# Sparse attention and two feed-forward layers on one core: the row maxima one tile later, their store between the transfers of a head, and two transfers issued by ScalarE

## The reference

```
scores = q @ k.T * (1 / sqrt(64))
thresh = max(scores, axis=-1) - tau
scores = where(scores >= thresh, scores, -1e9)
attn   = exp(scores - max(scores)) / (sum + 1e-9)
out    = attn @ v
# then x = (x @ w_a) * (x @ w_b) @ w_out; softmax-gated layer norm; @ w_out2
```

## Time and profile before

| | |
|---|---|
| median of 3 runs | 1073.68 us |
| the profiled execution | 1070.69 us, span 1068.4 us |
| attention with its prologue | about the first 388 us of the span |
| PE busy | 994.5 us (93%), 5844 matmuls |
| DVE, ACT, POOL busy | 534.7, 418.2, 251.7 us |
| PE waiting for the operands of `scores` | 49.2 us, 29 waits |
| `max_turn`: DVE waiting for POOL | 15.6 us, 16 waits |

### The profile page before, as it was taken

How to read it: one execution, slowest core, us unless ns; L and a number is a source line. 1 busy time by engine, 2 the same in 40 slices (tenths; PEclk the granted TensorE clock), 3 DMA queues, 4 the chain that set the end, 5 groups by cost and what they waited for, 6 DMA issues and landing times.

```text
span 1068.4 us, 16656 instructions
## 1 busy us (share of the span) xinstructions
PE 994.5 (93%) x5844; PEld 939.3 (88%) x5844; DVE 534.7 (50%) x863; ACT 418.2 (39%) x739; POOL 251.7 (24%) x242
## 2 busy tenths in 40 slices
PE   5789978888888889999999999999999999999998
PEld 5788878878888879999999999999999978888886
DVE  6666666666666575442122122222223485666564
ACT  2666666666666675331121121211212422322231
POOL 2656665665566670000000000000000000000000
PEclk9999999999999999999999999999999999999999
DMA  6554555555545425421001001000002200000000
GB/s 165 129 136 116 134 136 129 128 134 123 128 115 130 105 74 155 140 68 30 1 1 29 0 0 29 0 0 0 0 0 79 79 10 20 29 20 20 20 30 29
DMA packets 51566, 71.31 MB, mean 67 GB/s; under 512 B 14552, under 2 KB 24920, under 8 KB 51536
## 3 DMA queue, kind: packets, MB, share of 16 engines
q1 hardware_dynamic: 51536, 70.94, 25.2%
HBM read 33.25 MB, written 5.32 MB: 36 GB/s over the span
## 4 chain that ended last, share of the span: by engine, by line
PE 68%; SPq 9%; DMA 9%; issue 7%; DVE 3%; ACT 2%; POOL 1%; DVEq 0%; POOLq 0%; ACTq 0%
PE PS L1124 9%; PE PS L1125 9%; PE PS L1126 9%; DMA ops<-qk_lo 8%; PE PS L1195 5%; PE PS L1196 5%; PE PS L1194 5%; PE PS L1070 3%; PE PS L1253 3%; PE PS L1255 3%; PE PS L1254 3%; PE PS L1229 3%; PE PS L1227 3%; PE PS L1228 3%; PE PS L1072 2%
## 5 line engine op out<-in xcount | busy, mean ns | idle before, releaser
L1070 PE MATMUL PS<-ops 128*128 128x288 f32 x642 | 191.5, 318 | 63.3 <-DMA ops<-qk_lo 49.2
L528 POOL TENSOR_TENSOR p_lo<-prob,p_hi 128x576 fp32r<-128x576 f32 x144 | 207.3, 1440 | 135.9 <-ACT p_hi L607 130.2
L1070 PEld LDWEIGHTS PS<-ops 128*128 128x128 f32 x642 | 128.2, 200 | 78.0 <-issue 34.9
L1124 PE MATMUL PS<-x_hi,w_ab_rolled 128*128 128x384 f32 x576 | 192.5, 334 | 1.4 <-issue 1.4
L1126 PE MATMUL PS<-x_hi,w_ab_rolled 128*128 128x384 f32 x576 | 192.4, 334 | 0.0
L1125 PE MATMUL PS<-x_lo,w_ab_rolled 128*128 128x384 f32 x576 | 192.4, 334 | 0.0
L1072 PE MATMUL PS<-ops 128*128 128x288 f32 x642 | 184.3, 307 | 0.0
L944 DVE TENSOR_TENSOR gate<-gate,PS 128x384 f32<-128x384 f32 x72 | 39.9, 554 | 254.2 <-ACT gate L708 254.2
L827 DVE TENSOR_REDUCE neg_max<-PS 128x1 f32<-128x576 f32 x144 | 108.3, 754 | 107.9 <-PE PS L1072 107.8
L708 ACT ACTIVATE gate<-PS 128x384 f32<-128x384 f32 x72 | 35.5, 493 | 269.3 <-PE PS L1126 269.2
L600 ACT ACTIVATE prob<-PS 128x576 f32<-128x576 f32 x144 | 93.2, 647 | 94.6 <-PE PS L1072 91.7
(11 more groups left out here) (91 smaller groups left out, 1534.7 us busy)
## 6 DMA issues: line engine op xcount, KB each, us to landing
qk_raw<-qkT_dram SPq DMA_DIRECT2D x32, 288.0 KB, 3.1
ops<-qk_hi SPq DMA_DIRECT2D x62, 144.0 KB
ops<-qk_hi SPq DMA_DIRECT2D x31, 288.0 KB
ops<-qk_lo SPq DMA_DIRECT2D x62, 144.0 KB
v_raw<-v_tiles_dram SPq DMA_DIRECT2D x32, 160.0 KB, 2.8
xT<-head_sb SPq DMA_DIRECT2D x32, 144.0 KB, 3.1
out_dram<-o_sb SPq DMA_DIRECT2D x18, 256.0 KB, 2.0
stage<-inverse_dram SPq DMA_DIRECT2D x20, 192.0 KB, 3.9
```

The lines of the kernel that those rows point to most:

```text
L528: pool.tensor_tensor(p_lo[:, r, :], prob[:, s % RAW, :], p_hi[:, r, :].bitcast(F32), ALU.subtract).then_inc(p_lo_done, 1)
L1070: pe.matmul(ps[:, b, 0:HALF], weights[0][:, r, own], moving[0][:, r, cols], start=(n == 0), stop=False)
L1124: pe.matmul(bank, w[:, 0, :], x_hi[:, k, :], start=(k == 0), stop=False)
```

## The change

- `early_tile` gives tile s of the next pair in slot s: the maxima are nine tiles ahead, not ten. The `first` table places the groups of `values` of slots 3 to 6 anew, as `MID` of `scores` moves from slot 3 to slot 4.
- `high_max`, `low_max` and `turn_max` of the even head move from slot 4 to slot 5, those of the odd head from slot 8 to slot 0 of the next step. The prologue loses one tile and one turn.
- On SP `deal` is cut in two: `deal_first` (zeros and the high part of k) comes ahead of `store_max`, `deal_low` behind it. For the even head `load_v` now stands before `load_max`.
- The two transfers of the high part of q are issued by ACT (`deal_queries`): in slot 0, ahead of `exps`, for the next pair's odd head, and in slot 5 for the even head of the pair after.

```diff
         def early_tile(i, e, s):
-            return (*pair_at(i, e + 1), s + 1) if s + 1 < SLOTS else (*pair_at(i, e + 2), 0)
+            return (*pair_at(i, e + 1), s)
...
-            def deal(i, j):
+            def deal_first(i, j):
                 at_least(sp, st_done, number(i - 1, j // 2, MID + 1 if j % 2 == 0 else SLOTS))
                 if not (isinstance(i, int) and i == 0):
                     deal_zeros(i, j)
                 deal_high(i, j)
-                deal_low(i, j)
...
+                head(deal_first, i, e + 1, 1)
                 head(store_max, i, e, 1)
-                head(deal, i, e + 1, 1)
+                head(deal_low, i, e + 1, 1)
                 head(load_max, i, e, 1)
...
+                head(deal_first, i, e + 2, 0)
                 head(store_max, i, e + 1, 0)
-                head(deal, i, e + 2, 0)
+                head(deal_low, i, e + 2, 0)
+                head(load_v, i, e + 1, 1)
                 head(load_max, i, e + 1, 0)
-                head(load_v, i, e + 1, 1)
...
+            def deal_queries(i, j):
+                h, r = i * ROLL + j, j % ROLL
+                act.wait_ge(qk_hi_done, h + 1)
+                hi, o = qk_hi[:, j % 2, :].bitcast(F32), ops[:, 0, r, whole(r)].bitcast(F32)
+                act.dma_start(o[0:D, :], hi[0:D, :]).then_inc(ops_in[r], 16)
+                act.dma_start(o[D:P, :], hi[0:D, :]).then_inc(ops_in[r], 16)
...
-                    if s == MID and exists(ni, ne):
+                    if s == 0:
+                        high_max(i, 2 * e + 1)
+                        if exists(ni, ne):
+                            deal_queries(ni, 2 * ne + 1)
+                    if s == MID + 1 and exists(ni, ne):
                         high_max(ni, 2 * ne)
+                    if s == MID + 1 and exists(*pair_at(i, e + 2)):
+                        di, de = pair_at(i, e + 2)
+                        deal_queries(di, 2 * de)
                     if s == SLOTS - 1:
                         copy_head(i, 2 * e)
-                        if exists(ni, ne):
-                            high_max(ni, 2 * ne + 1)
...
-            first = {3: ((0, 0), (0, 1)), 4: ((0, 2), (1, 0)), 5: ((1, 1), (1, 2), (2, 0), (2, 1)),
-                     6: ((2, 2), (3, 0), (3, 1), (3, 2)), 7: ((4, 0), (4, 1), (4, 2))}
+            first = {3: ((0, 0), (0, 1), (0, 2), (1, 0)), 4: ((1, 1),), 5: ((1, 2), (2, 0), (2, 1), (2, 2)),
+                     6: ((3, 0), (3, 1), (3, 2)), 7: ((4, 0), (4, 1), (4, 2))}
```

More of the change, by code:

```diff
@@ L276, in exists, with whole @@
             return not isinstance(i, int) or 0 <= 2 * i + e < PAIRS
+        def whole(r):
+            return slice(REST * (r % 2), REST * (r % 2) + S)
         def number(i, e, s):
@@ L318, in load_v @@
                 sp.dma_start(v_raw[:, j % 2, :, :], v_tiles[h].rearrange("p (t d) -> p t d", d=D)).then_inc(v_in[j % 2], 16)
-            def whole(r):
-                return slice(REST * (r % 2), REST * (r % 2) + S)
             def deal_zeros(i, j):
@@ L325, in deal_zeros, with deal_high @@
                 sp.dma_start(ops[D:D + 2, 1, r, whole(r)].bitcast(F32), zeros[:, :]).then_inc(ops_in[r], 16)
-            def deal_high(i, j, split=qk_lo_done):
+            def deal_high(i, j, split=qk_lo_done, queries=False):
                 h, r = i * ROLL + j, j % ROLL
@@ L330, in deal_high @@
                 hi, o = qk_hi[:, j % 2, :].bitcast(F32), ops[:, :, r, whole(r)].bitcast(F32)
-                sp.dma_start(o[0:D, 0, :], hi[0:D, :]).then_inc(ops_in[r], 16)
-                sp.dma_start(o[D:P, 0, :], hi[0:D, :]).then_inc(ops_in[r], 16)
+                if queries:
+                    sp.dma_start(o[0:D, 0, :], hi[0:D, :]).then_inc(ops_in[r], 16)
+                    sp.dma_start(o[D:P, 0, :], hi[0:D, :]).then_inc(ops_in[r], 16)
                 sp.dma_start(o[0:D, 2:4, :], hi[D:P, :].rearrange("p (o s) -> p o s", o=1).to_broadcast([D, 2, S]))\
@@ L428, in _ @@
             load_qk(0, 2)
-            deal_high(0, 1, qk_hi_done)
+            deal_high(0, 1, qk_hi_done, True)
             deal_low(0, 1)
@@ L432, in _ @@
             load_v(0, 0)
-            deal_high(0, 2, qk_hi_done)
+            deal_high(0, 2, qk_hi_done, True)
             store_max(0, 0)
@@ L541, in step @@
                     ni, ne = pair_at(i, e + 1)
-                    if s == MID and exists(ni, ne):
+                    if s == 0:
+                        low_max(i, 2 * e + 1)
+                    if s == MID + 1 and exists(ni, ne):
                         low_max(ni, 2 * ne)
-                    if s == SLOTS - 1 and exists(ni, ne):
-                        low_max(ni, 2 * ne + 1)
                     if s == 1:
@@ L555, in _ @@
             low_max(0, 0)
-            low_max(0, 1)
             for e in range(2):
@@ L685, in _ @@
             high_qk(0, 3)
-            high_max(0, 1)
             last = heads // ROLL - 1
@@ L877, in step @@
                         mask(*pair_at(i, e - 1), SLOTS - 1)
-                    if s == MID and exists(ni, ne):
+                    if s == 0:
+                        turn_max(i, 2 * e + 1)
+                    if s == MID + 1 and exists(ni, ne):
                         turn_max(ni, 2 * ne)
-                    if s == SLOTS - 1 and exists(ni, ne):
-                        turn_max(ni, 2 * ne + 1)
                     mi, me = pair_at(i, e + 2)
@@ L918, in _ @@
                 score_max(0, 0, s, first_ps[s % 3])
-            score_max(0, 1, 0, first_ps[SLOTS % 3])
             dve.wait_ge(consts_in, 48)
@@ L923, in _ @@
             low_qk(0, 3)
-            turn_max(0, 1)
             last = heads // ROLL - 1
@@ L1163, in _ @@
                     product(first_ps[2], 0, MID, (qq, qx), (kk, kx), short_done, 1)
-            pe.wait_ge(max_done, SLOTS - 2)
-            scores(0, 1, 0, first_ps[SLOTS % 3])
             last = heads // ROLL - 1
```

## The result

The changed kernel takes 1019.5 us (median of 4 runs, 1016.82 to 1021.46) against 1074.03 us before: ratio 0.9495, 95% interval 0.9464 to 0.9525. The forecast was 1022 us with a range of 1010 to 1043. The profiled execution took 1021.25 us, its span 1019.1 us, 49.3 us less than the span before.

A forecast was written before the change was run, and what follows sets the result against it. A loop from the turn of the maxima through SP's issues to scores was taken as the bound. The period falling from 23.56 to 19.8 us, plus the ends, sums to 51.9 us saved: 1022 us predicted, range 1010 to 1043.

The forecast's parts named there:

- The bound: Attention: each head's scores wait for seven SP issues that start after another head's maxima are turned; 49.2 us in 29 waits.
- The floor and the even head: PE without waits needs 18.5 us a pair; even head's turn at T+5.4, store T+5.8, last low part issued T+7.25.
- The rival in which that load ends last: Even load of maxima lands at T4+12.6, PE waits 1.4 us more a pair in slot 0; 1040 us, 0.17 with late turn.
- 3.40 us of landing: Last low part of a head: time from issue to landing taken as the old 3.40 us, giving T+10.65 for the even head.
- better than the sum: Low parts land faster than 3.40 us and ACT's copy is early: period 19.1 us, 1013 us; chance 0.12.
- The stalls: New PE stalls each pair: 0.5 us at values (0, 0), 0.15 us at DVE in slot 8, 0.2 us more; 0.85 us.
- ACT's issues: Slots 5 and 0: two q issues stop ACT 1.15 us, moving slot 5's exponential to T4+4.8; 0.1 to 0.2 us lost.
- The loss in slot 7: Threshold of tile 5 ends at T4+7.0 while PE wants it at T4+6.9: 0.1 to 0.2 us lost.
- the slower rival: Each ACT stop is 3.6 us: period 24.6 us, 1087 us; decides from a stop of about 3.0 us; chance 0.03.
- The shared block: Skill's rule that sequencers share one locked descriptor block: ACT's slot 5 issues wait for SP's k, at most one issue.
- The end: End of attention: last odd wait with slow clock gains 1.5 us; maxima turned behind the scaling cost some 1.5 us once.
- Sum: Whole kernel: 48.9 us from 13 periods, 3.0 first pair, 1.5 last odd wait, less 1.5 at the end; 51.9 us.

The follow-up runs named there:

- e_conly: The kernel before with only ACT issuing the two transfers of the high part of q; tile and SP's order as before: 1039.3 us, ratio 0.9693.
- e_bonly: The kernel before with only SP's new order (store of the maxima between the deals), SP issuing q: 1033.5 us, ratio 0.9626.
- e_aonly: The kernel before with only the maxima nine tiles ahead, turned in slots 5 and 0: 1073.0 us, ratio 0.9999.
- e_tile: The changed kernel with the maxima ten tiles ahead again, turned in slots 4 and 8, and the old value groups: 1028.72 us, ratio 0.9595.
- e_copy: The changed kernel with ACT's copy of a head put ahead of the high part of the tile before it, slots 3 and 8: 1013.27 us, ratio 0.9456.
- e_sp: The changed kernel with the high part of q issued by SP again, ahead of the store of the maxima: 1017.22 us, ratio 0.9487.
- e_dbl: The changed kernel with two more issues on ACT at each stop, tiny transfers of zeros to unused memory: 1032.27 us.
- e_end: The changed kernel with the four loads of inverse sums moved behind the first deal of their step: 1016.96 us, ratio 0.9468.
- e_store: The changed kernel with the store of the maxima ahead of zeros, k and the low parts again: 1033.46 us, ratio 0.9647.

## Why the prediction was right

*The bound.* The loop from the turn of the maxima through SP's train to `scores` was it: shortening the train from either side brought 34 us (e_conly) or 39 us (e_bonly), and moving the turn with the deadline brought nothing (e_aonly).

*The floor and the even head.* The turn, store and last issue of the even head came 0.1 to 0.3 us earlier than worked out; those of the odd head, at 3.17, 3.57 and 4.82 us of slot 0, within 0.2 us. The wait of 0.2 us forecast for the low part did not come, nor the 0.15 us for the load of the maxima: it is issued at 177.85, and PE doesn't wait for it anywhere. The rival in which that load ends last had no trace. The 3.40 us of landing were carried over without a reason: with SP's new order e_bonly shows 2.45 to 2.54 us in most periods and e_tile 2.9 to 3.8. By any of these the part lands before slot 0, so nothing hung on it here. The rival "better than the sum" thus had one of its two conditions in e_bonly.

*The stalls.* This is the term that was mis-sized: 0.85 us forecast, about 1.5 us measured (20.08 less 140 matmuls by 0.1325, 18.55). I had the copy at slot 3, 0.5 us (0.53 measured), and missed that the other head's copy in slot 8 has the same place behind a high part, 0.65 us. e_copy shows both. The waits of 0.35 us that didn't come offset half of this: 19.8 forecast, 20.08 measured here and 20.01 in the mean.

*ACT's issues.* Their length was right (1.15 us). The exponential of slot 5 starts at 4.41 us of slot 4 (173.54; 4.8 forecast, 3.65 in e_sp), so ACT's issues delay it by some 0.76 us. But the threshold behind it starts at the same time with and without them (e_sp), held by the turn and the maximum that stand ahead of it on DVE. The loss in slot 7 is there (8 matmuls take 1.22 us at 175.49 where 1.06 is the work), and e_sp has it too (1.23 us at 174.54): it goes with the turn on DVE and not with ACT's issues, under which the prediction had booked it. The point from which the slower rival would decide was too near: e_dbl shows that of 3.0 us more a pair only 1.1 reach PE. The use of this part was not weighed at all: the sum would have been the same with SP issuing q, as e_sp has it.

*The shared block.* SP's issue of k at 172.15 (0.65 us) and ACT's of q at 172.22 and 172.76 (0.50, 0.62 us) run beside each other, about as long as SP's alone in the earlier trace rows. The Trainium skill's "Perfetto Trace Analysis", section "DMA Instruction — HWDGE (DVE, Sync)", would have one wait for the other. The rows of the changed kernel show no such wait: all 54 issues of ACT between 40 and 320 us overlap one of SP at least in part, and they take 0.47 to 0.51 us (the first of two) and 0.62 to 0.70 us. In e_conly the first takes 0.47 us with and without SP beside it. The second takes longer elsewhere, up to 0.92 us in e_conly and 0.94 us in e_tile (median 0.80); whether that is such a wait was not tried.

*The end.* I had 1.5 us of gain at the last odd wait and 1.5 us of loss behind the scaling. Neither came. The kernel before has both waits already:

```profile
359.84 0.37 PE L1070 MATMUL PS<-ops 128*128 128x288 f32 x1 [1.04 <-DMA ops<-qk_lo]
...
377.51 0.40 PE L1070 MATMUL PS<-ops 128*128 128x288 f32 x1 [2.60 <-DVE prob L841]
```

The first went from 1.04 to 1.48 us, with the slow clock behind it, because the loads of inverse sums are issued ahead of that deal (e_end). The second, for the threshold behind the scaling, went from 2.60 to 2.04 us, and PE waits nowhere for the maxima turned behind the scaling. That the two errors cancel is luck.

*Sum.* 51.9 us forecast, 54.5 us by the medians, 49.3 us by the two profiled spans (the profiled execution before was 3.3 us under its median, the one after 1.8 us over). The 13 periods gave 46.1 us by the spans, 48.9 forecast; all the rest 3.2 us, 3.0 forecast.

## What to carry to other kernels

Measure a wait for a transfer from the event that starts its chain to the event that needs it, and count what stands between on the issuing queue; parts of a change that shorten the same stretch don't add up (34 and 39 us alone, 44 us together without the tile), and a part that moves both ends brings nothing by itself but can make room for another (0 us alone, 16 us on top of the new order). Moving issues to a second engine is worth something only while the first is late. When the long waits go, look for the short ones that lay under them: here two copies of 0.7 us, then DVE's order, in which one operation waits for POOL. And a landing time holds for the order of transfers that it was measured in.

## What the runs showed of the hardware

How long the last low part takes to land depends on what is issued ahead of it. Where k and both low parts are issued in a row (the kernel before, e_aonly, e_store, e_conly) it landed in most periods 3.3 to 3.5 us after its issue began, whether q came from SP or from ACT; with the store between them (e_bonly) 2.45 to 2.54 us. Counted from the issue of k it is the same in both orders: 4.72 us in the earlier trace rows, 4.78 us in e_bonly (190.32 to 195.10). In e_tile, where ACT issues q beside and behind k, that is 5.5 to 6.6 us in most periods. What sets it was not tried.

An issue on ACT doesn't wait for the activations ahead of it in ACT's order: the first of q starts at 172.22, inside the high part from 171.99 to 172.67 and before the start, at 172.57, of the small activation that also stands ahead of it. The next exponential starts only after both issues.

DVE's subtraction for the low part of q and k became longer without a change to it, as the trace groups its 31 instances after (minimum, median and maximum in ns); before, the same three were 750, 1114 and 1295.

```profile
L833 DVE TENSOR_TENSOR qk_lo<-qk_raw,qk_hi x31: 748/1366/1716, 7.0 to 298.0; 128x576 fp32r<-128x576 f32 x31
```

It waits for POOL. In the period above POOL makes a low part of probabilities from 177.06 to 178.51; the subtraction starts inside it and ends at 179.13:

```profile
177.06 1.45 POOL L531 TENSOR_TENSOR p_lo<-prob,p_hi 128x576 fp32r<-128x576 f32 x1
```
```profile
177.61 1.52 DVE L833 TENSOR_TENSOR qk_lo<-qk_raw,qk_hi 128x576 fp32r<-128x576 f32 x1
```

In all 25 instances between 30 and 330 us of the kernel before, in all 54 of e_sp and e_copy, and in all of the changed kernel in which the trace shows POOL's operation by itself, the subtraction ends 0.60 to 0.63 us after the end of the POOL operation that was running when it started. So its length is what is left of POOL's operation, 0.2 to 1.1 us, and 0.6 us of its own. No run takes POOL's operation away from beside it.
